# Layer 1's columns from blocks of 128 rows instead of pairs of 96

## What is computed

```python
def _attn_ref(x, filt_r, filt_i):              # x: 2 x 3008 x 256
    X = np.fft.rfft(x, axis=1)
    Y = X * (filt_r + 1j * filt_i)[None, :, :]
    return np.fft.irfft(Y, n=x.shape[1], axis=1)

h = x @ moe_w_in                               # 6016 x 256 @ 256 x 2048
x = (np.maximum(h, 0) + moe_alpha * np.minimum(h, 0)) @ moe_w_out
h = np.maximum(x @ moe2_w_in, 0)
return (h * h) @ moe2_w_out                    # 6016 x 256
```

## Time and profile before

| | |
|---|---|
| median of 3 runs | 1121.08 us (1120.23 to 1121.08) |
| the profiled execution | 1121.51 us, with a span of 1119.7 us |
| TensorE matmuls busy | 1111.2 us (99%), 6997 |
| TensorE weight loads busy | 992.1 us (89%) |
| VectorE, ScalarE, GpSimd busy | 961.2, 662.5, 650.4 us |
| moved by DMA | 87.24 MB, mean 78 GB/s |

### The profile page before, as it was taken

One profiled execution on the slowest core, in us unless ns is written; L12 is line 12 of the kernel. 1 busy time (PEld: TensorE's weight loads), 2 busy tenths in 40 slices (PEclk: granted clock), 3 DMA queues, 4 the chain that ended last, 5 costly groups with the idle time before them and its releaser, 6 DMA issues.

```text
span 1119.7 us, 17393 instructions
## 1 busy us (share of the span) xinstructions
PE 1111.2 (99%) x6997; PEld 992.1 (89%) x6997; DVE 961.2 (86%) x1099; ACT 662.5 (59%) x785; POOL 650.4 (58%) x479
## 2 busy tenths in 40 slices
PE   9999999999999999999999999999999999999998
PEld 8568999898999989999898999999999999999997
DVE  4748899989988998898988888888898898888887
ACT  4956566766655555555555565555556555555653
POOL 0837587777856567666657455455455555555453
PEclk9999999999999999999999999999999999999999
DMA  9973225144120431312318600110110110110100
GB/s 213 276 222 85 68 67 134 34 111 133 40 78 1 137 97 59 110 49 89 110 60 297 228 23 14 38 34 4 37 37 1 37 38 1 38 38 1 38 19 19
DMA packets 56408, 87.24 MB, mean 78 GB/s; under 512 B 4712, under 2 KB 44168, under 8 KB 56328
## 3 DMA queue, kind: packets, MB, share of 16 engines
q1 hardware_dynamic: 56128, 85.98, 26.2%
q10 hardware_dynamic: 200, 0.15, 0.0%
HBM read 52.82 MB, written 33.29 MB: 77 GB/s over the span
## 4 chain that ended last, share of the span: by engine, by line
PE 88%; DVE 4%; DMA 2%; ACT 2%; issue 1%; POOL 1%; SPq 1%; DVEq 0%; ACTq 0%; POOLq 0%
PE bank L1102 15%; PE bank L1107 15%; PE bank L1103 14%; PE bank L1141 13%; PE bank L1128 13%; PE bank L1130 13%; PE bank L1080 3%; DMA filt_b<-filt 2%; DVE g_lo L898 1%; DVE g_raw L913 1%; PE bank L1000 1%; ACT filt_b L606 1%; PE bank L994 1%; DMA vc<-v_rows 0%; ACT t_hi_b L606 0%
## 5 line engine op out<-in xcount | busy, mean ns | idle before, releaser
L594 POOL TENSOR_TENSOR g_raw<-g_raw 128x250 f32<-128x250 f32 (+1 forms) x191 | 280.9, 1471 | 393.4 <-DVE g_raw L923 393.4
L898 DVE TENSOR_TENSOR g_lo<-g_raw,g_hi 128x1750 fp32r<-128x1750 f32 (+1 forms) x191 | 424.0, 2220 | 45.1 <-ACT g_hi L606 44.4
L732 ACT ACTIVATE g_raw<-bank 128x500 f32<-128x500 f32 (+1 forms) x384 | 226.2, 591 | 320.5 <-PE bank L1107 280.9
L606 ACT ACTIVATE g_hi<-g_raw 128x1750 fp32r<-128x1750 f32 (+1 forms) x191 | 318.9, 1670 | 50.4 <-POOL g_raw L597 48.8
L1130 PE MATMUL bank<-g_hi,w_lo 128*128 128x250 f32 (+1 forms) x1337 | 320.0, 279 | 0.0
L1128 PE MATMUL bank<-g_hi,w_hi 128*128 128x250 f32 (+1 forms) x1337 | 319.5, 279 | 0.0
L1102 PE MATMUL bank<-in_hi,w_hi 128*128 128x500 f32 (+1 forms) x768 | 302.3, 394 | 2.0 <-DVE g_raw L913 2.0
L1103 PE MATMUL bank<-in_hi,w_lo 128*128 128x500 f32 (+1 forms) x768 | 298.3, 388 | 0.0
L1130 PEld LDWEIGHTS bank<-g_hi,w_lo 128*128 128x128 f32 x1337 | 252.8, 189 | 7.5
L1128 PEld LDWEIGHTS bank<-g_hi,w_hi 128*128 128x128 f32 x1337 | 252.5, 189 | 7.4
L597 POOL TENSOR_TENSOR g_raw<-g_raw 128x250 f32<-128x250 f32 (+1 forms) x191 | 247.8, 1297 | 15.0
(11 more groups left out here) (87 smaller groups left out, 612.7 us busy)
## 6 DMA issues: line engine op xcount, KB each, us to landing
filt_b<-filt SPq DMA_DIRECT2D x36, 256.0 KB, 4.6
vc<-v_rows SPq DMA_DIRECT2D x22, 288.0 KB
v_rows<-v_out_b SPq DMA_DIRECT2D x24, 256.0 KB, 4.5
w_rows<-s_hi SPq DMA_DIRECT2D x8, 704.0 KB, 5.3
w_rows<-s_lo SPq DMA_DIRECT2D x8, 704.0 KB, 3.5
w_hi<-w_rows SPq DMA_DIRECT2D x8, 704.0 KB, 5.4
w_lo<-w_rows SPq DMA_DIRECT2D x8, 704.0 KB, 7.6
w_raw<-w SPq DMA_DIRECT2D x8, 512.0 KB, 8.7
```

Source lines behind the costliest of these rows:

```text
L594: pool.tensor_tensor(g_raw[:, r, T2, 0:h], g_raw[:, r, B22, 0:h], g_raw[:, r, T1N, 0:h], ALU.add).then_inc(t2_ready, 1)
L606: return act.activation(dst, src, ACT.Copy)
L732: act.activation(g_raw[:, r, 2 * j:2 * j + 2, 0:h], h_ps[j][:, 0:2 * h].rearrange("p (j d) -> p j d", j=2), ACT.Relu, scale=-1.0 if n < SL ...
L898: dve.tensor_tensor(g_lo[:, q, B11:T4 + 1, 0:h], g_raw[:, q, B11:T4 + 1, 0:h], g_hi[:, q, :, 0:h], ALU.subtract).then_inc(g_lo_ready, 1)
```

## The change

The rows of `v_rows` are stored in the order side, part, frequency: the constant of the inverse transform has its columns permuted, so that the partitions of `v_out` are (n2, c) and a group's rows are contiguous. For groups 1 to 11 the rows are then loaded in blocks of 128, without regard to sides, and a block's matmul writes the columns of every side that it touches. Where a block's border cuts a side, both blocks write its 47 columns and the bank adds them: only the first block of a half has the start flag. Blocks repeat after three (8 sides of 48 rows), so the constant has three forms, of 3, 4 and 3 sides: 141, 188 and 141 columns, 128 x 470 in all. A group has 528 or 576 rows: four blocks of 128 and one of 16 or 64. Its load is one DMA for the whole blocks and one for the rest. Group 0 keeps pairs of 96 rows and its loads in parts, with partitions in the new order.

```diff
+SIDES = 2 * WIDE
+BLOCKS = SIDES * HROWS // P
+BLOCK_SIDES = [(b * P // HROWS, -(-(b + 1) * P // HROWS)) for b in range(BLOCKS)]
+Y_AT = [sum(N1 * (e - a) for a, e in BLOCK_SIDES[:b]) for b in range(BLOCKS + 1)]
...
-        const_y_sb = sb(ctx, "const_y_sb", [ROWS, PAIR_TOK])
+        const_y_sb = sb(ctx, "const_y_sb", [P, Y_AT[BLOCKS]])
-        vc = sb(ctx, "vc", [ROWS, VC_PAIRS, DIM])
+        vc = sb(ctx, "vc", [P, VC_PAIRS, DIM])
+        first_rows = v_rows[0][0:VC_PAIRS * ROWS, :].rearrange("(j r) d -> r j d", r=ROWS)
...
             def load_vc(g):
                 sp.wait_ge(y_done, g * KD)
-                at, count = first_pair(g), pair_count(g)
-                for c in range(2):
-                    row = at * HROWS + c * SROWS
-                    sp.dma_start(vc[c * HROWS:(c + 1) * HROWS, 0:count, :],
-                                 v_rows[FIRST[g] // SEQ][row:row + count * HROWS, :]
-                                 .rearrange("(j r) d -> r j d", r=HROWS)).then_inc(vc_loaded, 16)
+                rows = side_count(g) * HROWS
+                src, full = v_rows[FIRST[g] // SEQ][first_side(g) * HROWS:first_side(g) * HROWS + rows, :], rows // P
+                sp.dma_start(vc[:, 0:full, :], src[0:full * P, :].rearrange("(b p) d -> p b d", p=P)
+                             ).then_inc(vc_loaded, 16)
+                sp.dma_start(vc[0:rows - full * P, full, :], src[full * P:rows, :]).then_inc(vc_loaded, 16)
...
+            def y_group(g):
+                at, lo, rows = FIRST[g] % SEQ, first_side(g), side_count(g) * HROWS
+                blocks = -(-rows // P)
+                pe.wait_ge(vc_loaded, 128 + 32 * g)
+                for half in range(KD):
+                    for b in range(blocks):
+                        depth, low = min(P, rows - b * P), b * P // HROWS
+                        begin = (lo + low) * N1
+                        t0 = max(at, begin)
+                        t1 = min(at + 2 * HALF[g], (lo - (-(b * P + depth) // HROWS)) * N1)
+                        col = Y_AT[b % BLOCKS] + t0 - begin
+                        mm = pe.matmul(y_ps[half][:, t0 - at:t1 - at], vc[0:depth, b, half * P:(half + 1) * P],
+                                       const_y_sb[0:depth, col:col + t1 - t0], start=(b == 0), stop=(b == blocks - 1),
+                                       skip_group_check=True)
                     mm.then_inc(y_done, 1)
...
+    inv = inv.reshape(P, 2, N2).transpose(0, 2, 1).reshape(P, P)
     turned = -np.concatenate([inv[N2:], inv[:N2]])
...
+    y = np.zeros((2, K1, N1))
+    y[0] = w * c1.T
+    y[1, 1:] = -(w * s1.T)[1:]
+    y = np.kron(np.eye(SIDES), y.reshape(HROWS, N1))
+    y = np.concatenate([y[b * P:(b + 1) * P, N1 * i:N1 * e] for b, (i, e) in enumerate(BLOCK_SIDES)], axis=1)
```

More of the change, by code:

```diff
@@ L88, with first_side, side_count @@
 PRIME = 4
[L91 to L96, removed]
+def first_side(g):
+    return (FIRST[g] % SEQ) // N1
+def side_count(g):
+    return -(-(FIRST[g] % SEQ + 2 * HALF[g]) // N1) - first_side(g)
 class Spectral:
@@ L377, in _, with load_vc_part @@
                     load_w1(n // 2)
[L379 to L386, removed]
+            def load_vc_part(at, rows, half):
+                sp.dma_start(vc[at:at + rows, :, half * P:(half + 1) * P], first_rows[at:at + rows, :, half * P:(half + 1) * P]
+                             ).then_inc(vc_loaded, 16)
             for n in range(B_UNITS):
@@ L398, in _ @@
                 elif n == VC_FIRST:
-                    for c in range(2):
[L401 to L404, removed]
-                                     .rearrange("(j r) d -> r j d", r=HROWS)).then_inc(vc_loaded, 16)
+                    for s in f0.v_stored:
+                        sp.wait_ge(s, 32)
+                    for side in range(2):
+                        load_vc_part(side * HROWS, HROWS, 0)
             for n in range(B_HALF, B_UNITS - 1):
                 sp.wait_ge(f0.v_stored[n % f0.vs], 48)
-            for c in range(2):
-                for side in range(2):
-                    load_vc_part(sp, c, side, 1, 0, B_HALF - 1, vc_loaded)
+            for part in range(4):
+                load_vc_part(part * K1, (B_HALF - 1) * WIDE, 1)
             sp.wait_ge(f0.v_stored[(B_UNITS - 1) % f0.vs], 48)
-            for side in range(2):
-                load_vc_part(sp, 0, side, 1, B_HALF - 1, 1, vc_loaded)
+            for part in range(2):
+                load_vc_part(part * K1 + (B_HALF - 1) * WIDE, WIDE, 1)
             store_ahead(0)
@@ L688, in _ @@
             act.wait_ge(f0.v_stored[(B_UNITS - 1) % f0.vs], 48)
[L689 to L694, removed]
+            for part in range(2, 4):
+                at = part * K1 + (B_HALF - 1) * WIDE
+                act.dma_start(vc[at:at + WIDE, :, P:2 * P], first_rows[at:at + WIDE, :, P:2 * P]
+                              ).then_inc(vc_last_loaded, 16)
             for u in range(AHEAD_PART[0], AHEAD_PART[1]):
@@ L1068, in _, with y_first @@
                 inverse_0(n)
[L1070 to L1081, removed]
+            def y_first(half):
+                pe.wait_ge(vc_loaded, 32 if half == 0 else 128)
+                if half == 1:
+                    pe.wait_ge(vc_last_loaded, 32)
+                for j in range(VC_PAIRS):
+                    a, b = j * PAIR_TOK, min(2 * HALF[0], (j + 1) * PAIR_TOK)
+                    mm = pe.matmul(y_ps[half][:, a:b], vc[0:ROWS, j, half * P:(half + 1) * P],
+                                   const_y_sb[0:ROWS, 0:b - a], start=True, stop=True)
+                mm.then_inc(y_done, 1)
+            def y_group(g):
[12 more added lines that the diff above has]
+                                       skip_group_check=True)
                     mm.then_inc(y_done, 1)
@@ L1146, in down_low @@
                     mm.then_inc(down_done, 1)
-            y_group(0, (0,))
+            y_first(0)
             for u in range(AHEAD_PART[0], AHEAD_PART[1]):
                 transform_ahead(u)
-            y_group(0, (1,))
+            y_first(1)
             for u in range(AHEAD_PART[1], AHEAD_PART[2]):
@@ L1266, in _constants @@
     sign = np.concatenate([-sign.T, sign.T]).astype(np.float32)
-    return blob, blob_1, full, y.reshape(ROWS, PAIR_TOK).astype(np.float32), sign, np.minimum(freq, SEQ - freq)
+    return blob, blob_1, full, y.astype(np.float32), sign, np.minimum(freq, SEQ - freq)
 def kernel(x, filt_r, filt_i, moe_w_in, moe_w_out, moe_alpha, moe2_w_in, moe2_w_out):
```

## The result

The changed kernel takes 1126.95 us (median of 6 runs, 1125.65 to 1131.15) against 1121.26 us: a ratio of 1.0054, interval 1.0044 to 1.0064, 5 to 7 us slower. The forecast was 1120.1 us, with a range to 1122.2. The highest run, 1131.15 us, is also the one with the lowest mean granted clock of TensorE, 0.997 against 0.999 to 1.000 in the others.

The account below looks back on a forecast made before the run. TensorE's own work was taken as the bound, busy 1111.2 of 1119.7 us. Passes -1.8 and constant +0.8 gave -1.0 us, so 1120.1 us from a median of 1121.08, range 1118.3 to 1122.2.

Parts of the forecast that it names:

- Fewer, wider passes: Column groups 1 to 11: 20 passes for 24, 2.48 us against 2.64 a group, saving 1.8 us in all.
- sign for groups of 2.7 us or more: Column groups in the chain: at 2.7 us or more, wide passes don't hide their weights and the price is wrong.
- D: Rival at the column passes: all 20 cost 0.110 us, 4.8 us saved, 0.8 paid, 1117.1 us; chance 0.03.
- Depth: Weight loads of column blocks: 128 rows instead of 96 counted as nothing; the 16-row rest costs a whole pass.
- The constant: Start: inverse-transform constant grows by 204,544 bytes on a full DMA queue, +0.8 us, bounds 0 and 1.1.
- no cover: Start: TensorE waits 0.36 and 0.33 us for x, so nothing was taken to hide the constant's 0.8 us.
- Loads, accumulation, group 0: Stored-row loads for later groups, adding into the bank, and group 0's partition order: each forecast to cost nothing.
- A: Rival after each group: VectorE's split or combination ends last, saving lost, only +0.8 remains, 1121.9 us; chance 0.10.
- B: Rival: VectorE and GpSimd collide more often on the chain, 1.7 us each, two give 1123.5 us; chance 0.07.
- C: Rival: one VectorE and GpSimd collision less on the chain, 1.7 us saved, 1118.4 us; chance 0.11.

Follow-up runs that it names:

- depth 96: Changed kernel with each group's rest read 96 partitions deep, extra partitions meeting zeros: 1120.42 us, 0.9995 of the kernel before; second set 1119.36 us, 0.9978.

## Why the prediction was wrong

*Fewer, wider passes: right.* A group was to take 2.48 us and save 0.16. Where the depth stays at 96 or more it takes 2.43 and saves 1.85/10 = 0.19. The trace of the changed kernel has its wide passes at the price too. The prediction's own sign for groups of 2.7 us or more was that wide passes don't hide their weights; the groups took 2.91 to 3.04, but it was the narrow rests, not the wide passes, whose weights were not hidden. The rival by which columns cost less (D) is wrong: groups would have taken 2.2 us.

*Depth: this is the step that failed.* It said that loads of 96 and 128 rows take 192 and 189 ns, "so I count nothing, and the 16-row rest costs a whole pass". The duration of the load was indeed no longer, 182 and 184 ns. What I didn't ask is whether it stays hidden. All passes of the kernel before are 96 or 128 rows deep; none was of 64 or fewer, so no row bounded the price, and instead of two ends I gave it a zero. A run of shallow passes costs 0.33 us in the traces, 7.3 us in 22 runs, four times the saving; by the ratios of the timed runs to depth 96 it is 6.6 and 8.5 us. With 7.3 in the sum, the saving at its measured 11 x 0.19 = 2.1 and the constant at nothing, 1121.1 - 2.1 + 7.3 = 1126.3 us, and 1126.95 was measured.

The Trainium skill has the rule (TensorEngine Tiling (Array Packing), section Tiling Modes): changing the tiling mode drains TensorE, and its modes are of 128, 64 and 32 rows. The runs agree with it in place, 80 rows free and 64 not, and give it a price. That a drain is the mechanism is the page's; the trace shows only starts further apart and loads without a lead. What happens inside TensorE at the switch stays open.

*The constant: not settled.* +0.8 us was forecast; alone it measures -0.4 to +1.5. In six traces with the constant of 235 KB at the start, group 0's columns began between 56.8 and 59.0 us, and in four without it between 57.5 and 58.2, so single executions vary by more than the term. My sentence that there was no cover, "TensorE has caught up with the DMA", rested on one execution.

*Loads, accumulation, group 0: right as far as seen.* No column pass after group 0 waits for rows, and adding into the bank is at the same spacing.

*The rivals.* A, B and C moved time between engines. The chain's shares of VectorE and GpSimd are as before, 4% and 1%, but one per cent is 11 us, too coarse for B's and C's 1.7. The steps from one group to the next say it: at depth 96 each of the ten is shorter than before by 0.17 to 0.20 us, about what its columns save, so nothing was taken away by another engine and no 1.7 us came or went there. In the changed kernel each is longer by 0.42 to 0.53. B was on the right side, but its mechanism had nothing to do with it.

## What to carry to other kernels

Fewer matmuls are only fewer if the next weights still load under the one before. Before a block size leaves a remainder, look at its contraction depth: keep it above 64 rows, beside deep passes, by padding to 80 or 96 with rows that meet zeros, which was free here, or put all shallow remainders next to one another. And when a change brings a shape that the trace of before does not hold, price it with a range, not with the duration of its nearest relative.

## What the runs showed that I had not expected

Besides the switch itself: TensorE's clock fell for some microseconds behind a group of columns in the profiled executions of the two kernels with shallow passes in the old layout. In the profiled executions of the other eight kernels every stretch of 10 us shows 1.00. In the timeline of the kernel with all passes shallow:

```profile
102.69 0.70 PE L1103 MATMUL bank<-in_hi,w_hi 128*128 128x504 f32 x1
103.19 0.62 PE L1104 MATMUL bank<-in_hi,w_lo 128*128 128x504 f32 x1
103.61 0.62 PE L1103 MATMUL bank<-in_hi,w_hi 128*128 128x504 f32 x1
104.03 0.62 PE L1104 MATMUL bank<-in_hi,w_lo 128*128 128x504 f32 x1
```

Passes of 504 columns start 0.42 us apart, not 0.23: that is the level of 1.2 GHz in place of 2.4. Directly before, TensorE had made 24 column passes of 64 rows. It happened behind group 1's and group 5's columns and not behind the other nine, so the shallow group is not enough by itself. Nor is it shown to be needed: single timed runs of kernels without any shallow pass have a low mean clock too (1125.26 us at 0.997 for the kernel before, 1125.88 at 0.995 for depth 96). But all four runs of this kernel have 0.997 or 0.998. What sets it off is open; no run here looks for it. It cost about 1.5 us each time (46.59 - 44.70 less the group's own 0.3). Of the changed kernel's timed runs the slowest has the lowest clock, 0.997.
